# A Fourier filter and two MLPs in one kernel: one pass over 376-token tiles against two passes over 512-token tiles with the Fourier stages batch by batch

## The reference

```
X = rfft(x, axis=1);  Y = X * (filt_r + 1j*filt_i);  y = irfft(Y, n=3008, axis=1)     # x: 4 x 3008 x 256
t = y.reshape(12032, 256)
t = relu(t @ w_in)**2 @ w_out                                                         # 256 -> 2048 -> 256
out = (silu(t @ w_gate) * (t @ w_val)) @ w_out2                                       # 256 -> 1536 -> 256
```

## Time and profile before

| | us |
|---|---|
| device time, median of 3 runs (2584.11 to 2586.1) | 2584.47 |
| span of the profiled execution, first to last instruction | 2579.7 |
| PE busy | 2486.1 (96%) |
| DVE busy | 1453.4 (56%) |
| ACT busy | 1072.8 (42%) |
| POOL busy | 179.6 (7%) |
| chain that ended last: share of PE | 89% |

### The profile page before, as it was taken

How to read it: one execution, slowest core, us unless ns; L and a number is a source line. 1 busy time by engine, 2 the same in 40 slices (tenths; PEclk the granted TensorE clock), 3 DMA queues, 4 the chain that set the end, 5 groups by cost and what they waited for, 6 DMA issues and landing times.

```text
span 2579.7 us, 43409 instructions
## 1 busy us (share of the span) xinstructions
PE 2486.1 (96%) x15344; PEld 2433.8 (94%) x15344; DVE 1453.4 (56%) x2582; ACT 1072.8 (42%) x2214; POOL 179.6 (7%) x145
## 2 busy tenths in 40 slices
PE   5686999999999999999999999999999999999998
PEld 3465999999999999999999999999999999999998
DVE  6498855555555555555555555555555555555554
ACT  3355733344444443334444443434444444334442
POOL 2296400000000000000000000000000000000000
PEclk8798999999999999999999999999999999999999
DMA  9765400000000000000000000000000000000000
GB/s 274 241 239 200 134 18 18 4 12 17 17 17 17 17 17 17 9 8 17 17 17 17 17 17 17 15 5 13 17 17 17 17 17 17 17 5 12 17 7 13
DMA packets 56717, 102.52 MB, mean 40 GB/s; under 512 B 6320, under 2 KB 32144, under 8 KB 55248
## 3 DMA queue, kind: packets, MB, share of 16 engines
q1 hardware_dynamic: 51168, 90.20, 11.0%
q0 software_dynamic: 5520, 11.95, 1.8%
HBM read 64.63 MB, written 37.49 MB: 40 GB/s over the span
## 4 chain that ended last, share of the span: by engine, by line
PE 89%; DVE 1%; DMA 1%; ACT 0%; issue 0%; POOL 0%; SPq 0%; ACTq 0%
PE psum L875 29%; PE psum L876 29%; PE psum L877 29%; PE psum L953 1%; PE psum L954 1%; DMA m_stage<-m_weights 0%; DVE g_lo L699 0%; DVE prod L816 0%; POOL m_lo L509 0%; DMA B_scratch<-b_out 0%; DMA b_in<-B_scratch 0%; DVE swish L793 0%; DVE y_lo L699 0%; ACT b_out L522 0%; DVE v_lo L699 0%
## 5 line engine op out<-in xcount | busy, mean ns | idle before, releaser
L875 PE MATMUL psum<-z_hi,m_hi 128*128 128x376 f32 x1536 | 513.6, 334 | 1.6 <-DVE z_lo L699 1.6
L832 DVE TENSOR_TENSOR swish<-psum,act_out 128x376 f32<-128x376 f32 x384 | 211.1, 550 | 536.2 <-ACT act_out L662 536.2
L876 PE MATMUL psum<-z_lo,m_hi 128*128 128x376 f32 x1536 | 512.4, 334 | 0.0
L877 PE MATMUL psum<-z_hi,m_lo 128*128 128x376 f32 x1536 | 511.8, 333 | 0.0
L662 ACT ACTIVATE act_out<-psum 128x376 f32<-128x376 f32 x384 | 185.6, 483 | 745.1 <-PE psum L877 745.1
L816 DVE SCALAR_TENSOR_TENSOR prod<-psum,act_out 128x376 f32<-128x376 f32 x512 | 281.4, 550 | 379.9 <-ACT act_out L643 372.5
L643 ACT ACTIVATE act_out<-psum 128x376 f32<-128x376 f32 x512 | 247.8, 484 | 438.7 <-PE psum L877 430.2
L875 PE MATMUL psum<-g_hi,m_hi 128*128 128x376 f32 x1024 | 345.6, 337 | 0.4 <-DVE g_lo L699 0.4
L875 PE MATMUL psum<-v_hi,m_hi 128*128 128x376 f32 x1024 | 341.9, 334 | 3.2 <-DVE v_lo L699 3.2
L876 PE MATMUL psum<-v_lo,m_hi 128*128 128x376 f32 x1024 | 342.6, 335 | 0.0
L877 PE MATMUL psum<-g_hi,m_lo 128*128 128x376 f32 x1024 | 342.4, 334 | 0.0
(11 more groups left out here) (72 smaller groups left out, 3647.6 us busy)
## 6 DMA issues: line engine op xcount, KB each, us to landing
a_in<-A_scratch SPq DMA_DIRECT2D x24, 512.0 KB, 4.9
b_in<-B_scratch SPq DMA_DIRECT2D x128, 96.0 KB
B_scratch<-b_out SPq DMA_DIRECT2D x23, 512.0 KB, 3.6
A_scratch<-a_out SPq DMA_DIRECT2D x15, 768.0 KB, 7.9
x_in<-x SPq DMA_DIRECT2D x16, 640.0 KB
w<-w_table POOLq DMA_DIRECT2D x32, 282.0 KB, 3.0
m_stage<-m_weights SPq DMA_DIRECT2D x34, 256.0 KB, 3.0
out<-o_out SPq DMA_DIRECT2D x64, 128.0 KB, 2.1
```

What stands on the lines that cost most here:

```text
L832: nc.vector.tensor_tensor(swish[f % 2][:, :], ring[2 * (f % 2)], act_out[f % 2][:, :], ALU.mult)\
L875: nc.tensor.matmul(dst, wh, vh, start=start, stop=False, skip_group_check=True)
L876: nc.tensor.matmul(dst, wh, vl, start=False, stop=False, skip_group_check=True)
L877: return nc.tensor.matmul(dst, wl, vh, start=False, stop=stop, skip_group_check=True)
```

## The change

The tile is 512 tokens wide (24 tiles, the last one 256). There are two passes: in the first all tiles go through the first MLP, whose result `z` goes to DRAM; in the second they are read back and go through the second MLP. Only batch 0 of the Fourier stages runs ahead of the MLPs. Those of batches 1 to 3 are set among the 384 steps of the first MLP: in a window of steps that starts at 0, 80 and 160, one of 16 S1 jobs in each of the steps 4 to 19, one of 12 S2 jobs in every third step from 28, its S3 job three steps later. S4 works on groups of 188 tokens (half as wide as a tile before), in two halves of channels, one half in an odd step. Each of these parts is now for one batch: S1's moving operand is 256 columns wide instead of 512, and an S2 or S3 job takes two values of `u` of one batch, 512 columns. POOL does no arithmetic any more. All loops are written out.

In `down2` the high and low halves of the weights lie side by side in SBUF, 512 columns; the high activations meet both at once (512 columns), the low ones only the high half (256 columns). The two halves of the sum are added after (`copy_low` on ACT, `add_out` on DVE).

```
-T = PI * Q                       # 376
+T = 512
+PAIR = 2
+STAGES = 3
...
+        HELD, HELD2 = 3, 2
+        WINDOW = [None, 0, 80, 160]
+        def s1_at(n):
+            for b in range(1, B):
+                i = n - WINDOW[b] - 4
+                if 0 <= i < PGS:
+                    return PGS * b + i
+            return None
+        def s2_at(n):
+            for b in range(1, B):
+                u, phase = divmod(n - WINDOW[b] - 28, 3)
+                if phase == 0 and 0 <= u < UPS:
+                    return UPS * b + u
+            return None
...
-            def load_x(c, k):
-                for q0, q1 in ((0, 80), (80, Q)):
-                    sp.dma_start(x_in[k][q0:q1, :, :, :], x_q[q0:q1, :, bass.ds(2 * c, 2), :])\
-                      .then_inc(x_loaded[k], 16)
+            def load_x(j):
+                b, i = divmod(j, PGS)
+                if j >= 4:
+                    sp.wait_ge(x_lo_done, j - 3)
+                sp.dma_start(x_in[j % 4][:, :, :],
+                             x[b].rearrange("(q p) d -> q p d", p=NP)[:, PAIR * i:PAIR * (i + 1), :])\
+                  .then_inc(x_loaded[j % 4], 16)
...
+            for j in range(PGS):                    # ahead of the MLPs, SP
+                if j + 4 < PGS:
+                    load_x(j + 4)
+                ...
+                store_a(j)
...
+            def s3(u, s4_jobs):
+                pe.wait_ge(y_lo_done, u + 1)
+                wait(pe, b_copied, u)
+                wait(pe, conv_done, s4_jobs)
+                transform(2, INV, y_hi[u % 2], y_lo[u % 2]).then_inc(inv_done, 1)
...
-                for n in range(OUT_GROUPS):
-                    tokens = slice(n * P, min(T, (n + 1) * P))
-                    last = product(acc2[n], (w_hi[f % 3][:, tokens], w_lo[f % 3][:, tokens]),
-                                   (w_out2(m2_hi, f), w_out2(m2_lo, f)), f == 0 and n != 1, f == NF2 - 1)
+                for k in range(OUT_GROUPS[t]):
+                    tokens = slice(k * P, (k + 1) * P)
+                    nc.tensor.matmul(psum[:, 4 + k, :], g_hi[n % 4][:, tokens], flat(m2_out[:, f, :, :]),
+                                     start=f == 0, stop=False, skip_group_check=True)
+                    last = nc.tensor.matmul(psum[:, 4 + k, 0:D], g_lo[n % 4][:, tokens], m2_out[:, f, 0, :],
+                                            start=False, stop=f == NF2 - 1, skip_group_check=True)
...
+            for n in range(STEPS):                  # the first pass, PE
+                up1(n)
+                j = s1_at(n)
+                if j is not None:
+                    s1(j)
+                u = s2_at(n)
+                if u is not None:
+                    s2(u)
+                job = s4_at(n)
+                if job is not None:
+                    s4(*job, s3_jobs)
+                    s4_jobs += 1
+                if n >= HELD:
+                    down1(n - HELD)
+                u = s2_at(n - 3)
+                if u is not None:
+                    s3(u, s4_jobs)
+                    s3_jobs += 1
+            for n in range(STEPS2):                 # the second pass, PE
+                up2(n)
+                if n < HELD:
+                    down1(STEPS - HELD + n)
+                if n >= HELD2:
+                    down2(n - HELD2)
```

More of the change, by code:

```diff
@@ L149, in build @@
         m1_lo, at = place(at, "m1_lo", [P, M1_PIECES, PIECE], F32R)
[L150 to L191, removed]
+        m1_end = at
         act_out, at = place_ring(at, "act_out", 2, [P, T])
@@ L310, in as_f32, with m2_at, flat, out_count @@
+        def m2_at(n):
+            w, phase = divmod(n - M2_FROM, M2_PERIOD)
+            return w if phase == 0 and 0 <= w < M2_PIECES else None
         def as_f32(tile_ap):
             return tile_ap.bitcast(F32)
+        def flat(tile_ap):
+            return tile_ap.rearrange("p a b -> p (a b)")
+        def out_count(k, tiles):
+            n = 0
+            for t in range(k, tiles, 2):
+                first, last = T * t, T * t + WIDTH[t]
+                cuts = {*range(first, last, P)} | {c for c in range(0, last, Q) if c >= first}
+                n += 16 * len(cuts)
+            return n
@@ new lines, in copy_low @@
+            def copy_low(t, half):
+                act.wait_ge(w_used, NF2 * (t + 1))
+                if t:
+                    act.wait_ge(o_done, sum(OUT_GROUPS[:t - 1]) // 2 + half + 1)
+                copy(o_low[:, 2 * half:2 * half + 2, :], psum[:, 4 + 2 * half:6 + 2 * half, D:])\
+                    .then_inc(o_low_done, 1)
+            for j in range(PGS):
+                high_x(j)
+                if j:
+                    copy_a(j - 1)
+                if j >= PGS - STAGES:
+                    high_m1(j - PGS + STAGES)
@@ L696, in _ @@
+            high_w(STEPS2 - 1)
+            for half in range(OUT_GROUPS[TILES - 1] // 2):
+                copy_low(TILES - 1, half)
         @block.vector
@@ L870, in _ @@
+            low_w(STEPS2 - 1)
+            for half in range(OUT_GROUPS[TILES - 1] // 2):
+                add_out(TILES - 1, half)
         @block.tensor
@@ L895, in _ @@
-            s1_chunk(0, True)
-            with pe.Fori(1, NCHUNK // 2) as i:
-                s1_chunk(i, False)
-            def transform(matrix, bank, hi, lo, first_half=None):
-                for h in range(NHALF):
-                    cols = slice(h * HALF, (h + 1) * HALF)
-                    last = product(psum[:, bank + h, :], (w23[:, matrix, 0, :], w23[:, matrix, 1, :]),
-                                   (hi[:, cols], lo[:, cols]), True, True)
-                    if first_half is not None and h == 0:
-                        last.then_inc(first_half, 1)
-                return last
@@ L1068, in pieces @@
+            for n in range(STEPS2):
+                up2(n)
[3 more added lines that the diff above has]
+                    down2(n - HELD2)
+            for n in range(STEPS2 - HELD2, STEPS2):
+                down2(n)
 def pieces(*matrices):
```

1286 lines of the change are left out of this document (681 added, 605 removed).

## The result

| | before | after |
|---|---|---|
| device time, median, us | 2584.29 (4 runs, 2582.36 to 2586.1) | 2655.29 (4 runs, 2653.61 to 2657.15) |
| after over before, with its 95% interval | | 1.0279 [1.0264, 1.0293] |
| span of the profiled execution | 2579.7 | 2651.8 |
| first matmul of the first MLP | 259.71 | 174.32 |
| first matmul of the second pass | | 1463.21 |

What follows compares the result with a forecast made beforehand. Before: about 260 us of Fourier stages with PE half idle, then 2320 us set by matmul count times step. Forecast: 178 + 2196.1 + 107.9 + 54.2 + 44 + 13 + 16 = 2609.2, with 4.8 2614 us; range 2530 to 2675.

Steps and rivals of the forecast that it cites:

- The front, 178: Fourier stages of batch 0 alone, before the first MLP: 178 us instead of 259.7, bounds 155 to 210.
- The packet count's reading: Small-packet count of the earlier profile: a 94-row DMA goes to two engines, so a load of `x` takes 4.0 us.
- The loads of `x` among the steps, +44: S1 steps of the first pass: loads at 5.2 us a job outlast steps of 3.45, +44 us, bounds 0 and 119.
- the prediction's own last sentence: Forecast is wrong if the first pass begins before 150 us or the windows show no wait for `x`.
- Rival 1: Loads of `x` spread over four or more engines and don't bind: 2525 us, 2.3% faster; chance 0.20.
- Rival 2: PE's clock falls to 1.2 GHz in the windows, 48 steps of 6.4 us: +58, 2672 us; chance 0.13.
- DVE and ACT hide beneath: MLP steps: two DVE operations of about 0.69 us and two of ACT fit under a first-pass step of 2.74.
- S3 behind S4: First pass: 11 of 36 S3 jobs wait for an S4 half of the same step, about 1.2 us each, +13.
- The MLP matmuls, -58: Both MLPs: same columns in 3888 fewer matmuls, 0.2285 us per 512 columns; 2196.1 us against 2253.2.
- Rival 3: Wider matmuls buy less: 0.233 us at 512 columns, +39, 2653 us; chance 0.07.
- S4's pairs: S4 matmul pairs among the first-pass steps: 244 at 0.222 us, 54.2 us against 55.1 before.
- the rest: 16 us: 11.7 as before, 3 for last stores and two more operations, 1 at the change of passes.

## Why the forecast was right or wrong, point by point

- **Direction: right; size: wrong.** Slower, as forecast with a chance of 0.68, and the measured time is within the range, but by 71 us instead of 30.
- **The front, 178: right as a sum** (174.3), with terms that were off and partly cancel. The packet count's reading, two engines for 94 rows, is confirmed to the packet by the two cuts. S1 ends at 90 as forecast, but not at the pace of the loads, 4.0 us: most of its jobs follow by 4.7, and ACT waits mainly for the stores to land, as in the windows. Its waits up to 92 us:

```profile
ACT a_out L572 <- DMA A_scratch<-a_out: 48.1, 12, 10.2
ACT x_hi L572 <- DMA x_in<-x: 16.7, 4, 5.5
```

These pieces of the chain of waits answer to the earlier trace rows; the last job's store lands at 90.08 and S2 starts at 94.25, where I had 99. From there S2 and S3 take 58.5 us instead of 55, and the way through `B_scratch` and S4 to the first `v_hi` 21.6 instead of 24:

```profile
88.06 2.02 DMA A_scratch<-a_out
90.15 2.62 DMA a_in<-A_scratch
92.79 0.64 ACT a_hi L572
93.45 0.70 DVE a_lo L783
94.25 0.77 PE psum L1001
```

- **The loads of `x` among the steps, +44: right in place and size** (47.6 in the S1 steps, of which 42.1 go with the split; by windows 20.1, 13.7 and 13.9 where 18.7, 12.7 and 12.7 were summed), half wrong in how. I looked for ACT or DVE waiting for `x_in`, and by the prediction's own last sentence its absence would have spoken against the forecast. ACT waits instead for the store of `a_out`, and in the first window for pieces of the MLP weights, which stand in the same queue; the split removes both waits. So the loads are the cause, though nothing waits for them by name.
- **Rival 1, `x` spread over more engines: false**, by the packets and by the run of 47 + 47 rows. With the cut of 80 + 14 its two gains appear, the first `v_hi` at 133.0 (178 - 45) and 5.5 us lost in the S1 steps; the time is 2571.4 and not its 2525, because the S2 loss and the second pass remain.
- **Rival 2, the clock in the windows: false.** In these stretches of the kernel after, with the S1 steps of the first two windows, the granted clock (the last but two) is 0.98, so 2.4 GHz for nearly all of the time (1.00 in the third, from 773 to 856 us):

```profile
184.00:262.00 78.00, 62.31 (x316) 50.51 (x316) 45.28 (x82) 45.09 (x96) 8.20 (x16) 0.98 0.45 136
476.00:559.00 83.00, 73.97 (x371) 60.04 (x370) 45.10 (x84) 45.83 (x98) 8.21 (x16) 0.98 0.34 104
```

- **The step that failed: "DVE and ACT hide beneath".** It was weighed with a mean: two operations of 0.69 us in a step of 2.74. That holds for 204 of the 384 steps, which lose 2 us in all. It was never asked for the steps into which the Fourier jobs were moved, where DVE also has two filter products, a sum and two low parts: 5.3 us of DVE without a pause, with PE's next operand at the end. PE then waits 1.1 us, 33 times. The forecast did see that those steps lose something and gave S3 behind S4 the blame, 13 us. The run with `a_lo` earlier shows 41 us for DVE's order and leaves 6.6 for S3 behind S4. The two together, 47.8 against 13, are 34.8 of the 42.6 us by which the span was missed.
- **The MLP matmuls, -58 (by the sum's own terms 2253.2 - 2196.1 = 57.1): right in kind, mis-sized in the second pass.** In the first pass a wide step is 0.2275 us, where I took 0.2285: 4.7 us less. In the second it comes to about 0.2314 (4.173 less four narrow ones at 0.1178, by 16), and the pass takes 1181.2 instead of 1164.4. Of these 16.8 us the step makes 276 x (4.173 - 4.127) = 12.7; 2.1 are three narrow `down1` steps that I had put in the first pass (18 x 0.1178), 2.0 lie in its first three steps and behind its last wide one. I had carried the step from S2 and S3 to operands that lie elsewhere. 7.1 us go with the region's place; the work of DVE and ACT is ruled out; the other 5.6 of the step are open.
- **Rival 3, width buys less: false as a mechanism.** Its step of 0.233 is near the second pass, but the first pass, of the same width, has 0.2275, and the narrow `down2` costs 11.3 us more. By an estimate from the figure of the Trainium skill ("TensorE: Matmul & The Clock Gate", section "Wait — 56ns, not 53.3ns?"), 2.5 ns a matmul, it would have been 2.8; the trace shows 10 ns a matmul and disagrees.
- **S4's pairs and the rest.** I counted a pair at 0.222 us; two of them take 0.38 here, 7.8 us less for 244 pairs, but the steps with S4 alone lose 12.2: together +4.4, which no run took apart. Most of these steps lose 0.09; three, one in each window, lose 1.1, and it stays open why. Behind the last matmul there are 7.4 us instead of the 16 that I kept for all the rest.

The ledger of the first pass: S2 and S3 +34.8, loads of `x` +3.6, S4 +4.4, all other steps +2.2, the wide step of 0.2275 instead of 0.2285 -4.7, the three narrow `down1` steps that belong to the second -2.1: +38.2 of the 38.1 measured. With the second pass's +16.8, the front's -3.7 and the end's -8.6 that is the 42.6 us.

## What to carry to other kernels

When work is moved among the steps of a loop, write out the order of each engine for the step that gets it (each does its operations in the order in which the kernel issues them), up to the operation that TensorE waits for next; a busy share, here 61% of DVE, says nothing on that. Look at each DMA's row count when a transfer is cut anew: the same bytes cost 84 us more in one piece of 94 rows than as 80 and 14, and others' stores in the same queue pay as well. Where PE never waits, time the step of a matmul at the place where it will stand, since the step depends on where the operands lie.

## What the hardware showed that I had not expected

- The place of operands in SBUF changes a matmul's step with no other change: 4.173 to 4.147 us for a step of 20 matmuls when the region of its weights moved by 640 bytes, 1181.2 to 1174.1 us over the pass, in both runs that have the edit. At one and the same width, 512 columns, the mean step was 0.2275 us in the first pass and about 0.2314 in the second.
- Loads that few DMA engines share hold up a transfer of another shape in the same queue: the store of 96 rows landed after 2.3 us with `x` in 80 + 14 rows, 8.3 with 94 and 12.4 with 47 + 47, its own size the same.
